# Adding the second half of each token tile's rows with an accumulating transfer instead of on VectorE

## The reference

```
X = fft(x, axis=1); X = fft(X, axis=2); x = X.real            # 2 x 3008 x 256
x = x.reshape(6016, 256)
x = (sigmoid(x @ w_gate) * (x @ w_val)) @ w_out               # 256 -> 1536 -> 256
h = x @ w_in;  y = (h * cos(h)) @ w_out2                      # 256 -> 2048 -> 256
```

## Time and profile before

| | us |
|---|---|
| median of 3 runs (lowest, highest) | 952.49 (952.25, 952.51) |
| the profiled execution's own time | 952.45 |
| its span | 950.6 |
| TensorE busy in the span | 944.0 (99%) |
| VectorE busy | 748.5 (79%) |
| ScalarE busy | 598.0 (63%) |
| GpSimd busy | 652.1 (69%) |

### The profile page before, as it was taken

The page is one execution under the profiler, slowest core; times in us unless marked ns, Lnnn a source line. Parts: engine busy times, 40 slices in busy tenths (PEclk is TensorE's granted clock), DMA queues, the critical chain, the costliest instruction groups (busy, mean ns, idle before and its releaser), DMA issues.

```text
span 950.6 us, 14429 instructions
## 1 busy us (share of the span) xinstructions
PE 944.0 (99%) x4177; PEld 778.6 (82%) x4177; DVE 748.5 (79%) x1158; ACT 598.0 (63%) x1076; POOL 652.1 (69%) x527
## 2 busy tenths in 40 slices
PE   9999999999999999999999999999999999999998
PEld 7888888888888888888888888888888888888886
DVE  7989988888888988998766767667676667667666
ACT  7565455544554554555677677777767767767765
POOL 3138778889888789799476666756656665765552
PEclk9999999999999999999999999999999999999999
DMA  9940011211210300303700200110020011001001
GB/s 375 335 127 7 33 45 45 84 44 44 83 61 26 126 33 32 116 27 123 269 1 0 83 5 1 45 44 1 1 87 1 1 44 44 1 1 45 1 0 44
DMA packets 24265, 59.01 MB, mean 62 GB/s; under 512 B 7818, under 2 KB 14610, under 8 KB 23442
## 3 DMA queue, kind: packets, MB, share of 16 engines
q1 hardware_dynamic: 22628, 51.10, 14.9%
q0 software_dynamic: 1440, 7.02, 1.9%
q10 hardware_dynamic: 144, 0.26, 0.1%
HBM read 38.14 MB, written 20.24 MB: 61 GB/s over the span
## 4 chain that ended last, share of the span: by engine, by line
PE 91%; DVE 1%; issue 0%; ACT 0%; DVEq 0%; ACTq 0%
PE bank L1275 24%; PE bank L1213 19%; PE bank L1295 9%; PE bank L1297 9%; PE bank L1296 9%; PE bank L1248 7%; PE bank L1249 7%; PE bank L1250 7%; DVE gv L994 0%; DVE val L935 0%; DVE bank L1032 0%; DVE gl L998 0%; DVE yo L1060 0%; DVE rem L986 0%; ACT sn L702 0%
## 5 line engine op out<-in xcount | busy, mean ns | idle before, releaser
L435 POOL TENSOR_TENSOR gl<-gv,gh 128x502 fp32r<-128x502 f32 x189 | 241.4, 1289 | 183.6 <-ACT gh L710 183.6
L417 POOL TENSOR_TENSOR al<-act_,ah 128x502 fp32r<-128x502 f32 x144 | 191.9, 1353 | 4.8 <-ACT ah L616 4.7
L994 DVE TENSOR_TENSOR gv<-sn,bank 128x502 f32<-128x502 f32 x192 | 129.8, 676 | 50.8 <-ACT sn L702 48.5
L986 DVE SCALAR_TENSOR_TENSOR rem<-rnd,bank 128x502 f32<-128x502 int32 x192 | 125.5, 674 | 55.7 <-ACT rnd L695 55.1
L710 ACT ACTIVATE gh<-gv 128x502 fp32r<-128x502 f32 x192 | 118.5, 617 | 80.9 <-DVE gv L994 80.6
L412 POOL TENSOR_TENSOR act_<-gate,val 128x502 f32<-128x502 f32 x72 | 114.1, 1584 | 59.3 <-DVE val L935 56.0
L616 ACT ACTIVATE ah<-act_ 128x502 fp32r<-128x502 f32 x144 | 89.5, 625 | 101.0 <-PE bank L1250 50.3
L702 ACT ACTIVATE sn<-rem 128x502 f32<-128x502 f32 x192 | 119.0, 620 | 52.5 <-DVE rem L986 52.5
L1295 PE MATMUL bank<-gh,wo 128*128 128x502 f32 x384 | 150.1, 391 | 0.1
L1297 PE MATMUL bank<-gh,wo 128*128 128x502 f32 x384 | 149.7, 390 | 0.0
L1296 PE MATMUL bank<-gl,wo 128*128 128x502 f32 x384 | 149.6, 389 | 0.0
(11 more groups left out here) (160 smaller groups left out, 1746.6 us busy)
## 6 DMA issues: line engine op xcount, KB each, us to landing
xin<-xq SPq DMA_DIRECT2D x6, 1032.0 KB, 7.9
x_d<-xr SPq DMA_DIRECT2D x6, 1004.0 KB, 3.8
xr<-x_d SPq DMA_DIRECT2D x6, 1004.0 KB, 4.8
out<-yo SPq DMA_DIRECT2D x10, 502.0 KB, 2.8
tev<-tev_d POOLq DMA_DIRECT2D x6, 756.0 KB, 10.3
wo_d<-wot SPq DMA_DIRECT2D x8, 512.0 KB, 2.6
wo<-wo_d SPq DMA_DIRECT2D x8, 512.0 KB, 4.5
w_d<-w2t SPq DMA_DIRECT2D x4, 896.0 KB, 4.6
```

The source lines that it names most:

```text
L417: nc.gpsimd.tensor_tensor(al[:, f % 2, s, :], act_[:, s, :], ah[:, f % 2, s, :].bitcast(F32), ALU.subtract).then_inc(a_lo, 1)
L435: nc.gpsimd.tensor_tensor(gl[:, e, :], gv[:, e, :], gh[:, e, :].bitcast(F32), ALU.subtract).then_inc(g_lo, 1)
L994: nc.vector.tensor_tensor(gv[:, e, :], sn[:, e % 2, :], bank_of(q, (C11, C12, C22, CHAIN)[e]), ALU.mult).then_inc(gvs, 1)
```

## The change

The host lays out `xq` so that quarters 0, 1 and quarters 2, 3 of a tile are two blocks of 128 x 1032 floats. SP's queue loads the first block into the tile's buffer. GpSimd waits for its landing and then issues the second block as a transfer with `accum_op=ALU.add` onto the same bytes (`add_x`). `fold_cols` waits for that transfer. `fold_rows` and its semaphore go. A buffer is half as large, so there are four in the same place, and a load waits only from `i` = 4 on, for `fold_cols(i-4)`. SP's wait for `mid_d` goes, and so does GpSimd's wait for `sums` ahead of the fourth `tev` transfer. GpSimd's issues now stand in the order x0, todd0, x1, todd1, x2, todd2, x3, tev0, tev1, tev2, x4, tev3, x5, tev4, tev5 (x for an accumulating transfer).

```diff
-XN = 2 * 4 * ROW
+XN = 2 * 2 * ROW
-    xin = put("xin", R, [2, 2, 4, ROW])
+    xin = put("xin", R, [4, 2, 2, ROW])
         def load_x(i):
-            if i >= 2:
-                sp.wait_ge(fold_o, i - 1)
-            sp.dma_start(xin[:, i % 2, ...], xq[i]).then_inc(x_in[i % 2], 16)
+            if i >= 4:
+                sp.wait_ge(fold_o, i - 3)
+            sp.dma_start(xin[:, i % 4, ...], xq[i, 0]).then_inc(x_in[i % 4], 16)
...
-        load_x(3)
-        sp.wait_ge(mid_d, 3)
-        load_x(4)
-        load_x(5)
+        for i in range(3, XT):
+            load_x(i)
...
-        for m, (done, count) in enumerate(((x_in[0], 16), (x_in[1], 16), (x_in[0], 32))):
-            pool.wait_ge(done, count)
+        def add_x(i):
+            pool.wait_ge(x_in[i % 4], 16 * (i // 4) + 16)
+            pool.dma_start(xin[:, i % 4, ...], xq[i, 1], accum_op=ALU.add).then_inc(x_all[i % 4], 16)
+
+        for m in range(M):
+            add_x(m)
             pool.dma_start(todd[:, m, ...], todd_in[m]).then_inc(odd_in[m], 16)
+        add_x(M)
         for i in range(2 * M):
             if i == M:
                 pool.wait_ge(w_lo, 4)
-                pool.wait_ge(sums, 4)
             pool.dma_start(tev[:, i // M, i % M, ...], tev_in[i]).then_inc(ev_in[i], 16)
+            if i in (2, 3):
+                add_x(i + 2)
...
-        def fold_rows(i):
-            xv = xin[:, i % 2, :, :, :]
-            dve.wait_ge(x_in[i % 2], 16 * (i // 2) + 16)
-            nc.vector.tensor_tensor(xv[:, :, 0:2, :], xv[:, :, 0:2, :], xv[:, :, 2:4, :], ALU.add).then_inc(sums, 1)
         def fold_cols(i):
-            dve.wait_ge(sums, i + 1)
+            dve.wait_ge(x_all[i % 4], 16 * (i // 4) + 16)
```

More of the change, by code:

```diff
@@ L153, in build @@
     d_in, id_in, w_in = sem("d_in"), sem("id_in"), [sem(f"w_in{i}") for i in range(4)]
-    x_in = [sem("x_in0"), sem("x_in1")]
+    x_in, x_all = [sem(f"x_in{i}") for i in range(4)], [sem(f"x_all{i}") for i in range(4)]
     odd_in, ev_in = [sem(f"odd_in{m}") for m in range(M)], [sem(f"ev_in{i}") for i in range(2 * M)]
@@ L158, in build @@
     w_done, w_rest, wt_hi, wt_lo = (sem(n) for n in ("w_done", "w_rest", "wt_hi", "wt_lo"))
-    sums, fold_e, fold_o, seq_s, seq_d = (sem(n) for n in ("sums", "fold_e", "fold_o", "seq_s", "seq_d"))
+    fold_e, fold_o, seq_s, seq_d = (sem(n) for n in ("fold_e", "fold_o", "seq_s", "seq_d"))
     mid_s, mid_d, xo_hi, xo_lo, xe_hi, xe_lo = (sem(n) for n in ("mid_s", "mid_d", "xo_hi", "xo_lo", "xe_hi", "xe_lo"))
@@ L193, in load_x @@
         def load_x(i):
-            if i >= 2:
-                sp.wait_ge(fold_o, i - 1)
-            sp.dma_start(xin[:, i % 2, :, :, :].rearrange("p d q n -> p (d q n)"), xq[i]).then_inc(x_in[i % 2], 16)
+            if i >= 4:
+                sp.wait_ge(fold_o, i - 3)
+            sp.dma_start(xin[:, i % 4, :, :, :].rearrange("p d q n -> p (d q n)"), xq[i, 0]).then_inc(x_in[i % 4], 16)
         def load_o1(i):
@@ L365, in _ @@
             pool.wait_ge(blank, 1 + i)
-        for m, (done, count) in enumerate(((x_in[0], 16), (x_in[1], 16), (x_in[0], 32))):
-            pool.wait_ge(done, count)
+        def add_x(i):
+            pool.wait_ge(x_in[i % 4], 16 * (i // 4) + 16)
+            pool.dma_start(xin[:, i % 4, :, :, :].rearrange("p d q n -> p (d q n)"), xq[i, 1], accum_op=ALU.add).then_inc(x_all[i % 4], 16)
+        for m in range(M):
+            add_x(m)
             pool.dma_start(todd[:, m, :, :, :].rearrange("p c s n -> p (c s n)"), todd_in[m]).then_inc(odd_in[m], 16)
+        add_x(M)
         for i in range(2 * M):
@@ L774, in split_w @@
             nc.vector.tensor_tensor(wl[i % 2], wraw[i % 4][:, :], wh[i % 2].bitcast(F32), ALU.subtract).then_inc(w_lo, 1)
-        def fold_rows(i):
-            xv = xin[:, i % 2, :, :, :]
-            dve.wait_ge(x_in[i % 2], 16 * (i // 2) + 16)
-            nc.vector.tensor_tensor(xv[:, :, 0:2, :], xv[:, :, 0:2, :], xv[:, :, 2:4, :], ALU.add).then_inc(sums, 1)
         def fold_cols(i):
-            xv = xin[:, i % 2, :, :, :]
-            dve.wait_ge(sums, i + 1)
+            xv = xin[:, i % 4, :, :, :]
+            dve.wait_ge(x_all[i % 4], 16 * (i // 4) + 16)
             if i:
@@ L786, in fold_cols @@
                 dve.wait_ge(seq_d, i)
-            nc.vector.tensor_tensor(tt[:, :, :, 0:P], xv[:, :, 0:2, 0:P], xv[:, :, 0:2, HROW:HROW + P], ALU.add).then_inc(fold_e, 1)
-            nc.vector.tensor_tensor(tt[:, :, :, P:2 * P], xv[:, :, 0:2, 1:HROW], xv[:, :, 0:2, HROW + 1:ROW], ALU.subtract).then_inc(fold_o, 1)
+            nc.vector.tensor_tensor(tt[:, :, :, 0:P], xv[:, :, :, 0:P], xv[:, :, :, HROW:HROW + P], ALU.add).then_inc(fold_e, 1)
+            nc.vector.tensor_tensor(tt[:, :, :, P:2 * P], xv[:, :, :, 1:HROW], xv[:, :, :, HROW + 1:ROW], ALU.subtract).then_inc(fold_o, 1)
         def fold_half(i):
@@ L848, in _ @@
         split_w(1)
-        fold_rows(0)
         fold_cols(0)
@@ L855, in _ @@
         odd_x_lo(0)
-        fold_rows(1)
         even_x_lo(0)
@@ L862, in _ @@
         odd_x_lo(1)
-        fold_rows(2)
         split_w(5)
@@ L869, in _ @@
         odd_x_lo(2)
-        fold_rows(3)
         even_x_lo(2)
@@ L877, in _ @@
         fold_quarter(3)
-        fold_rows(4)
         even_x_lo(3)
@@ L883, in _ @@
         odd_x_lo(4)
-        fold_rows(5)
         even_x_lo(4)
@@ L1378 @@
         xq[:, :, :, :, q, P], xq[:, :, :, :, q, ROW - 1] = ((nyq, pad) if q % 2 == 0 else (pad, nyq))[0][..., q], ((nyq, pad) if q % 2 == 0 else (pad, nyq))[1][..., q]
-    xq = xq.reshape(XT, P, XN)
+    xq = np.ascontiguousarray(xq.reshape(XT, P, 2, 2, 2, ROW).transpose(0, 3, 1, 2, 4, 5)).reshape(XT, 2, P, XN)
     w1 = np.concatenate([moe_w_gate, moe_w_val], axis=1).reshape(HALVES, P, WCH, WCOL)
```

## The result

The changed kernel took 960.56 us (median of 4 runs, 959.95 to 961.04) against 952.39 us for the kernel before beside it: a ratio of 1.0084, 95% interval 1.0071 to 1.0096, slower by 8.2 us. The profiled execution has a span of 959.0 us against 950.6.

The account below looks back on a forecast made before the run. TensorE was taken to bound the kernel. Stall +5.7, clock +2.5, less 0.8 of old idle gave +7.4 us on 952.45: 959.9 us, own range 958.0 to 962.5 (chance 0.45), 8 in 10 range 955.6 to 968.0.

Parts of the forecast that it names:

- What bounds, and that `turn(2)` has no slack against `split_w(2)`: TensorE bounds, busy 944.0 of 950.6 us; at 13 us each us of later `split_w(2)` on VectorE delays `turn(2)` one us.
- The landing: Tile 0's accumulating transfer ahead of `fold_cols(0)`: issued at 8.5, 7.7 us to landing, so landing at 16.2.
- The stall: TensorE ahead of `turn(2)` in the opening: start moves 5.7 us, to 18.7; ends put at 2.5 and 10.5 us.
- The clock: Matmuls after TensorE's idle stretch, from `turn(2)`, run at the lower level: 2.5 us, bounds 0 and 2.5.
- What comes back: Of 1.11 us of old TensorE idle in the fourth and fifth windows, 0.8 us is given back.
- The later tiles at nothing, the cover thin: Tiles after tile 0 and `tev` transfers: nothing put down; cover gone if an accumulation costs four times its bytes.
- The removed waits and GpSimd's issues at nothing: SP's and GpSimd's removed waits priced at nothing; GpSimd's six more issues, 0.53 us each, fall in its idle time.
- the clock did not hold: Rival: same stall at `turn(2)`, but TensorE comes back at the upper clock level: 957.4 us, chance 0.25.
- the accumulation was not four times as dear: Rival: accumulation four times its bytes or row by row, tile 0 landing at 21 or later: 965 to 985 us, chance 0.18.
- the landing of the 64 KB row (4.5 us): Not-slower rival: tile 0's accumulating transfer has only its fixed part, landing at 13.0 or before: 953.9 us, chance 0.05.

Follow-up runs that it names:

- in quiet: Changed kernel plus six transfers behind all its work, each waited for alone: plain 516 KB landed in 3.4 and 3.6 us, accumulating 5.4 and 5.6.

## Why the prediction was right, point by point

- *What bounds, and that `turn(2)` has no slack against `split_w(2)`*: right. Every us of the late fold went to TensorE at that place.
- *The landing*: forecast 7.7 us after an issue at 8.5, measured 9.6 after 8.55. The term was mis-sized by 1.9 us. I had put the two prices, once the bytes (6.5) and twice the bytes (8.7), on a line through two old rows. In the runs the plain transfer took 7.2 and the accumulating one 9.6: twice the bytes was the right end, and both lay 0.7 to 0.9 above the line. The stall was 7.7 us for 5.7.
- *The clock*: forecast 2.5 us, measured 2.3, near the top of its bounds, as nearly the whole of `turn(2)` ran at the lower pace. In the runs with a shorter stall fewer matmuls were slow. The granted clock did show it, at 0.50, which the prediction could not see from the opening of the kernel before.
- *What comes back*: forecast 0.8, measured 1.7. I had taken the idle time as span less busy time, and the busy time of TensorE overstates its work, since the ends of matmuls are modelled. The starts of like instructions in the two traces say it rightly: from the same point in front of the even tables' matmuls to the `odd_tile` behind them it is 5.20 us before (39.07 to 44.27) and 3.78 after (48.86 to 52.64), which is 1.4 of the 1.7.
- *The later tiles at nothing, the cover thin*: this step stood in the sum at zero and was right there, but by 0.6 us only. The prediction put the cover's end at an accumulation of four times its bytes; at twice the bytes it was all but used up. It had the last `tev` landing near 50, in place of 42.5, and TensorE wanting the fifth at 51. Measured, the fifth landed at 50.8 (42.9 before) and the last at 52.8 (44.8 before), and TensorE began on the fifth at about 51.4: the prediction had given the last transfer the fifth's place. For tile 1 it had a landing at 21 to 23.4 and VectorE there at 23.0; it landed at 24.3, and VectorE came at 26.4, late by tile 0's landing and by 1.3 us of waiting for ScalarE, so no wait came of it. What the prediction did not see is what this means: with tile 0's stall taken away, the loss stays (959.3 us). The stall was the loss that showed; the DMA engines were a second one of nearly the same size beneath it.
- *The removed waits and GpSimd's issues at nothing*: right, and shown. That GpSimd would stand 17.4 us for room for its transfers the prediction did not see; the larger descriptor area shows that this cost nothing.
- *The rivals*: the clock did not hold; the accumulation was not four times as dear; the landing of the 64 KB row (4.5 us) is not reached even in quiet by 516 KB added (5.4). The fit of the Trainium skill's page "DMA: Bandwidth & Descriptors", section "Anatomy of one DMA — SWDGE (gpsimd) path", gives 3.2 us for a plain 516 KB; in quiet that took 3.4 to 3.6, so it nearly agrees there, and it is short by 4 in company. The rule of the Trainium skill's page "Collectives: The Full Stack", section "Why ReduceScatter is half of AllGather", that an add reads two sources and halves the rate agrees with the factor of two in engine time measured here.

The time of 960.56 against 959.9 is closer than its terms: the stall was 2.0 us too small and what comes back 0.9 too small, of opposite sign. That part of the closeness is luck.

No version here beats the kernel before. The experiments point away from the idea in this stage: every addition handed to a transfer saves 1.14 us of VectorE, which does not bound, and takes 1.35 us (8.1 / 6) from the DMA engines, which do, until 42 us.

## What to carry to other kernels

Before work is moved from a compute engine to the DMA engines, look at the DMA share of that very stage: at 1.0 it is a bound as hard as TensorE's, even where no wait for a transfer is longer than 0.6 us. Price an accumulating transfer at twice its bytes and one more landing behind the plain one. And where a stall is found, ask what would be late if it went: here taking away either of two losses gave back about 1 us of 8.

## What the runs showed of the hardware

An accumulating transfer took the DMA engines about twice the time of a plain one with the same bytes (2.0 times in the opening, 1.9 to 2.2 in quiet). GpSimd's rows read 0.88 to 0.91 us for the issue of one, but the plain issue right behind it began 0.56 to 0.58 us later and reads 0.87 to 0.90 too; among plain issues both figures were 0.53, so the addition cost GpSimd little. With 1024 bytes of descriptor area GpSimd stood still from the fifth of these transfers on, 17.4 us in all, which 1536 bytes ended. Behind 8.1 us without a matmul TensorE's granted clock was 0.50, and it was back at 1.00 about 5 us after the work began again. With other idle stretches it took less: 2.7 us behind 5.2 us with plain transfers, 3.2 us behind 2.9 us with tile 0 on VectorE. The last wait alone did not decide: behind the wait for the fifth `tev` the clock stayed at 1.00 after 2.34 us in one kernel and was at 0.50 after 2.37 us in another.
